# Fill and gate splits of a fused attention and mixture-of-experts kernel: relu and scale of the sums' input on ScalarE, constant rows shared out by engine, the gate splits one operation a step

## What is computed

```python
# attention: 2 batches, 8 heads, 576 positions, 64 columns a head
scores = scale * q @ k.T
cum = cumsum(maximum(s, 0))                    # s: one value per position and head
scores = where(causal, -1e9, scores + minimum(-(cum_i - cum_j), 0))
attn = exp(scores - max(scores)); attn /= sum(attn) + 1e-9
x = attn @ v                                   # then 1152 tokens of 512 values
logits = x @ w_gate; noise_scale = log1p(exp(x @ w_noise))   # stage 2: choose 2 of 8
out[mask] += weight * (maximum(x[mask] @ w1[e], 0) @ w2[e])
P = exp(x @ moe2_w_gate - max); 8 rounds of balancing        # stage 3: all 8 experts, dense
out += P[:, e] * (maximum(x @ w1[e], 0) @ w2[e])
```

## Time and profile before

| what | us |
|---|---|
| median of 3 runs (lowest to highest) | 1201.5 (1199.59 to 1203.03) |
| the profiled execution | 1204.84 |
| its span, from first to last instruction | 1203.1 |
| mean granted clock of TensorE in it | 0.993 |

### The profile page before, as it was taken

How to read it: one execution, slowest core, us unless ns; L and a number is a source line. 1 busy time by engine, 2 the same in 40 slices (tenths; PEclk the granted TensorE clock), 3 DMA queues, 4 the chain that set the end, 5 groups by cost and what they waited for, 6 DMA issues and landing times.

```text
span 1203.1 us, 20068 instructions
## 1 busy us (share of the span) xinstructions
PE 1188.2 (99%) x7085; PEld 1062.0 (88%) x7085; DVE 697.3 (58%) x1584; ACT 426.4 (35%) x918; POOL 254.8 (21%) x303
## 2 busy tenths in 40 slices
PE   8999999999999999999999999999999999999998
PEld 6999888888888888889889899899899898898997
DVE  6664775554444451657566575575574675665753
ACT  7675344444344241224123232242241241332320
POOL 8767111111111456201001011011010010110110
PEclk9998999999999999999999999999999999999999
DMA  7770654444455420013120220210211201202102
GB/s 179 182 173 4 246 179 153 155 150 153 180 180 203 161 61 1 1 36 106 36 71 6 64 70 0 70 40 30 70 35 35 70 24 46 70 0 70 35 1 78
DMA packets 40230, 102.81 MB, mean 85 GB/s; under 512 B 4750, under 2 KB 23694, under 8 KB 38010
## 3 DMA queue, kind: packets, MB, share of 16 engines
q1 hardware_dynamic: 33722, 85.70, 22.7%
q0 software_dynamic: 3360, 11.01, 3.0%
q10 hardware_dynamic: 3104, 5.54, 1.4%
HBM read 87.82 MB, written 10.30 MB: 82 GB/s over the span
## 4 chain that ended last, share of the span: by engine, by line
PE 95%; DVE 2%; ACT 1%; DMA 1%; issue 1%; POOL 0%; DVEq 0%; POOLq 0%
PE bank L1164 10%; PE bank L1163 10%; PE bank L1162 9%; PE bank L1118 9%; PE bank L1116 9%; PE bank L1117 9%; PE bank L940 5%; PE bank L942 5%; PE bank L941 5%; PE bank L922 5%; PE bank L924 4%; PE bank L923 4%; PE bank L847 3%; PE bank L828 1%; PE bank L792 1%; PE bank L829 1%
## 5 line engine op out<-in xcount | busy, mean ns | idle before, releaser
L1164 PE MATMUL bank<-part2h,partl 128*128 128x512 f32 x504 | 198.6, 394 | 0.0
L1163 PE MATMUL bank<-part2l,parth 128*128 128x512 f32 x504 | 197.6, 392 | 0.0
L761 POOL TENSOR_TENSOR part2l<-raw_part,part2h 128x512 fp32r<-128x512 f32 x56 | 72.4, 1293 | 589.9 <-ACT part2h L1414 589.9
L1162 PE MATMUL bank<-part2h,parth 128*128 128x512 f32 x504 | 195.7, 388 | 0.0
L1886 DVE SCALAR_TENSOR_TENSOR x_sb<-bank,share_now,x_sb 128x512 f32<-128x512 f32 x126 | 94.1, 747 | 159.5 <-PE bank L1164 159.5
L1118 PE MATMUL bank<-x_forms,forml 128*128 128x288 f32 x448 | 132.1, 295 | 0.0
L1116 PE MATMUL bank<-x_forms,formh 128*128 128x288 f32 x448 | 131.9, 294 | 0.0
L1117 PE MATMUL bank<-x_forms,formh 128*128 128x288 f32 x448 | 131.8, 294 | 0.0
L1565 DVE SCALAR_TENSOR_TENSOR hl<-bank,hh 128x336 fp32r<-128x336 f32 (+1 forms) x88 | 45.7, 519 | 131.5 <-ACT hh L1291 131.3
L922 PE MATMUL bank<-xTh,w1h 128*128 128x336 f32 (+1 forms) x352 | 115.9, 329 | 0.7 <-DVE xTl L1545 0.5
L923 PE MATMUL bank<-xTl,w1h 128*128 128x336 f32 (+1 forms) x352 | 113.9, 324 | 0.0
(11 more groups left out here) (244 smaller groups left out, 2464.2 us busy)
## 6 DMA issues: line engine op xcount, KB each, us to landing
raw<-in_w SPq DMA_DIRECT2D x15, 2048.0 KB, 7.7
raw_part<-in_w1b SPq DMA_DIRECT2D x14, 1024.0 KB, 6.0
raw_part<-in_w2b SPq DMA_DIRECT2D x14, 1024.0 KB, 6.1
k_raw<-in_kT SPq DMA_DIRECT2D x16, 288.0 KB, 5.3
y_dram<-x_sb ACTq DMA_DIRECT2D x16, 256.0 KB, 4.4
q_raw<-in_qT SPq DMA_DIRECT2D x8, 288.0 KB, 5.0
q_two<-w2l SPq DMA_DIRECT2D x8, 288.0 KB, 5.8
x_dram<-x_sb SPq DMA_DIRECT2D x1, 2304.0 KB, 9.2
```

The lines of the kernel that those rows point to most:

```text
L1162: pe.matmul(dst, parth[:, l, ts], part2h[:, l, :], start=(l == 0), stop=False)
L1163: pe.matmul(dst, parth[:, l, ts], part2l[:, l, :], start=False, stop=False)
L1164: mm = pe.matmul(dst, partl[:, l, ts], part2h[:, l, :], start=False, stop=(l == FL - 1))
```

## The change

- Sums' input: relu and scale move from DVE (line 1455) to ACT, right behind the rounding of the identity; DVE's scan waits for a new semaphore `s_positive`.
- Constant rows: POOL fills the first two slots of k_top, and all of q_top's second, for whose ones it waits until ACT has written q_top's first; ACT writes q_top's first only. The third slots are filled by DVE inside its loop, half a slot a step in steps 0 to 3, and the two rows of ones in step 4. POOL's memset in step 4 is gone.
- `rinv`'s first filling on DVE moves from ahead of the sums to step -1.
- Fillers on PE: five of 256 columns instead of three of 512 ahead of the loop, and 128 columns instead of 256 in the nine steps before step -4.
- Gate splits: the six operations of step 60 are spread over steps 57, 58, 59, 62, 63 and 64.

```diff
-        WARM_UPS = 3
+        WARM_UPS = 5
...
-        W1_LOW_AT, EARLY_AT, GATES_AT = ALL - 4 * DC, ALL - ST, 60
+        W1_LOW_AT, EARLY_AT, GATES_AT = ALL - 4 * DC, ALL - ST, (57, 58, 59, 62, 63, 64)
...
-            for w in range(HEADS_RING):
+            for w in range(2):
                 pool.memset(k_top[w][HD:P, :].bitcast(F32), 1.0).then_inc(aug_ready, 1)
-            pool.memset(q_top[2][HD:P, :].bitcast(F32), 0.0).then_inc(q_rows_clear, 1)
+            pool.memset(q_top[1][HD:P, :].bitcast(F32), 0.0).then_inc(q_rows_clear, 1)
+            pool.wait_ge(q_rows_clear, 1)
+            pool.wait_ge(q_rows_ready, 1)
+            pool.memset(q_top[1][HD:HD + 2, :].bitcast(F32), 1.0).then_inc(q_rows_ready, 1)
...
             for k in range(-LOW_AHEAD, ALL):
-                if k == LAST_ROWS_AT:
-                    pool.wait_ge(q_rows_clear, 1)
-                    pool.wait_ge(q_rows_ready, 2)
-                    pool.memset(q_top[2][HD:HD + 2, :].bitcast(F32), 1.0).then_inc(q_rows_ready, 1)
...
             for _ in range(WARM_UPS):
-                keep_warm(BANK)
+                keep_warm(BANK // 2)
             for k in range(-ROUGH_AHEAD, ALL):
                 if k + ROUGH_AHEAD < ALL:
                     rough(k + ROUGH_AHEAD)
                 if k < 0:
-                    keep_warm(BANK // 2 if k < -SCORES_AHEAD else P)
+                    keep_warm(P)
...
             act.copy(ident_r[:], ident[:]).then_inc(ident_rounded, 1)
+            act.wait_ge(s_loaded, 32)
+            act.activation(cum_p[0:CUM_END, :], cum_s[0:CUM_END, :], ACT.Relu, scale=SQRT_D).then_inc(s_positive, 1)
             act.wait_ge(const_ready, 6)
             act.wait_ge(first_rows, 1)
-            for w in range(2):
-                act.activation(q_top[w][HD:P, 0:S], causal[HD:P, 0:S], ACT.Relu, bias=row_ones[HD:P, 0:1], scale=0.0)
-                act.activation(q_top[w][HD:P, S:N], causal[HD:P, 0:S], ACT.Relu, bias=row_ones[HD:P, 0:1], scale=0.0).then_inc(q_rows_ready, 1)
+            act.activation(q_top[0][HD:P, 0:S], causal[HD:P, 0:S], ACT.Relu, bias=row_ones[HD:P, 0:1], scale=0.0)
+            act.activation(q_top[0][HD:P, S:N], causal[HD:P, 0:S], ACT.Relu, bias=row_ones[HD:P, 0:1], scale=0.0).then_inc(q_rows_ready, 1)
...
-            link(v.tensor_copy(rinv[:].rearrange("p a b -> p (a b)"), ones[:, 0:2 * STEPS]))
-            v.wait_ge(s_loaded, 32)
-            link(v.tensor_scalar(cum_p[0:CUM_END, :], cum_s[0:CUM_END, :], 0.0, SQRT_D, ALU.max, ALU.mult))
+            v.wait_ge(s_positive, 1)
...
-            def split_gates():
-                v.wait_ge(gates_loaded, 48)
-                for which, (cn, c0, g0) in enumerate(((2 * E, 0, 0), (E, 2 * E, 4 * E))):
-                    high, low = gate_w[:, :, g0:g0 + cn], gate_w[:, :, g0 + cn:g0 + 2 * cn]
+            def split_gates(step):
+                which, part = divmod(step, 3)
+                cn, c0, g0 = ((2 * E, 0, 0), (E, 2 * E, 4 * E))[which]
+                high, low = gate_w[:, :, g0:g0 + cn], gate_w[:, :, g0 + cn:g0 + 2 * cn]
+                if step == 0:
+                    v.wait_ge(gates_loaded, 48)
+                if part == 0:
                     link(v.tensor_copy(high, gates[:, :, c0:c0 + cn]))
+                elif part == 1:
                     link(v.tensor_tensor(low, gates[:, :, c0:c0 + cn], high.bitcast(F32), ALU.subtract))
-
+                else:
                     link(v.tensor_tensor(fold[which][:], ident[0:2 * cn, 0:cn], ident[0:2 * cn, cn:2 * cn], ALU.add))
...
+            def last_rows(k):
+                cols = slice(k % 2 * S, (k % 2 + 1) * S)
+                if k == 0:
+                    v.wait_ge(aug_ready, 3)
+                if k < 2:
+                    ones_row = v.memset(k_top[2][HD:P, cols].bitcast(F32), 1.0)
+                    if k == 1:
+                        ones_row.then_inc(aug_ready, 1)
+                elif k < 4:
+                    link(v.memset(q_top[2][HD:P, cols].bitcast(F32), 0.0))
+                else:
+                    v.wait_ge(q_rows_ready, 2)
+                    v.memset(q_top[2][HD:HD + 2, :].bitcast(F32), 1.0).then_inc(q_rows_ready, 1)
...
-                if k == GATES_AT:
-                    split_gates()
+                if k == -1:
+                    link(v.tensor_copy(rinv[:].rearrange("p a b -> p (a b)"), ones[:, 0:2 * STEPS]))
+                if 0 <= k < STEPS:
+                    last_rows(k)
+                if k in GATES_AT:
+                    split_gates(GATES_AT.index(k))
```

More of the change, by code:

```diff
@@ L204, in build @@
         s_loaded = sem("s_loaded")
+        s_positive = sem("s_positive")
         cum_summed = sem("cum_summed")
@@ L388, in build @@
         CUM_ROWS = slice(FIRST_ROWS, CUM_END)
-        SECOND_LATER, LAST_ROWS_AT = 2, 4
+        SECOND_LATER = 2
         FIRST_LOWS = (0, 1, 4, 5, 2, 3, 6, 7)
@@ L1516, in token_low @@
                                 xTh[:, :, ts].bitcast(F32), ALU.subtract).then_inc(st.xTl_ready, 1)
-            def split_gates():
-                v.wait_ge(gates_loaded, 48)
-                for which, (cn, c0, g0) in enumerate(((2 * E, 0, 0), (E, 2 * E, 4 * E))):
-                    high, low = gate_w[:, :, g0:g0 + cn], gate_w[:, :, g0 + cn:g0 + 2 * cn]
+            def split_gates(step):
[5 more added lines that the diff above has]
+                if part == 0:
                     link(v.tensor_copy(high, gates[:, :, c0:c0 + cn]))
+                elif part == 1:
                     link(v.tensor_tensor(low, gates[:, :, c0:c0 + cn], high.bitcast(F32), ALU.subtract))
+                else:
                     link(v.tensor_tensor(fold[which][:], ident[0:2 * cn, 0:cn], ident[0:2 * cn, cn:2 * cn], ALU.add))
-                assert count[0] == GATES_SPLIT, count[0]
+                assert step < 5 or count[0] == GATES_SPLIT, count[0]
+            def last_rows(k):
[11 more added lines that the diff above has]
+                    v.memset(q_top[2][HD:HD + 2, :].bitcast(F32), 1.0).then_inc(q_rows_ready, 1)
             for k in range(-ROUGH_AHEAD, ALL):
@@ L1908, in _ @@
             far_half(E - 2, 1, False)
-GATES_SPLIT = 5 + 6
+GATES_SPLIT = 6 + 6
 def kernel(q, k, v, s, moe_w_gate, moe_w_noise, moe_noise, moe_w1, moe_w2, moe2_w_gate, moe2_w1, moe2_w2):
```

## The result

| kernel | median of the runs (lowest to highest), us | profiled execution, us | its span | mean granted clock in it |
|---|---|---|---|---|
| before | 1200.62 (1198.13 to 1207.29), 22 runs | 1204.84 | 1203.1 | 0.993 |
| changed | 1205.63 (1203.02 to 1208.98), 22 runs | 1203.89 | 1202.2 | 0.994 |

The changed kernel is slower by the ratio 1.0035, with a 95% interval of 1.0024 to 1.0046, which is 4.2 us (2.9 to 5.5). The forecast was 1197.1 us, faster by 4.4. The time lies above the stated range.

The account below looks back on a forecast made before the run. TensorE (PE), busy in 99% of the span, was taken to bound the kernel. From a median of 1201.5 us, 0.9 (fill), 1.1 (gate stall) and 2.4 (half the low-clock spell) were taken off, giving 1197.1; range 1194.2 to 1201.3.

Parts of the forecast that it names:

- SP's new wait: SP's queue: load_cum(2) waits for k_top's third slot until about 20, double_k(2) behind it; cost 0, at worst 1 us.
- DVE's memsets: DVE in steps 0 to 4: half a slot 0.6 us, two rows 1.2; cost 0, each maximum having over 1 us of cover.
- The sign that was named: Steps 0 to 7: the prediction is wrong if PE waits for DVE there.
- The sums' input: Fill: relu on ACT at 3.1 lets the first rough product start at 7.5 instead of 9.10, 1.6 us earlier.
- How much of it lasts: Fill: rough(5) starts some 0.5 us earlier, not 1.6, its small row standing behind the last load and landing at 12.1.
- The fillers: From rough(5) to the first scores: four fillers shrink, by at most 0.9 us; 0.4 taken.
- rival (c): Fill: PE's 1.5 us wait ahead of rough(5) drops the clock, costing 4.8 us; time 1204.3 to 1206, chance 0.07.
- The gate splits: Around 97 us: spreading them removes PE's full stall of 1.09 us, bounds 0.6 and 1.3.
- The sum: Whole kernel: median 1201.5 - 0.9 - 1.1 - 2.4 = 1197.1 us, for the fill, gate stall and half the low-clock spell.
- rival (b): Transfer queue eats the fill's gain, SP's and DVE's waits take 0.3, gate stall gives 0.8; 1201.0 us, chance 0.08.

Follow-up runs that it names:

- e12: Changed kernel with SP's load of head 2's sums' rows moved behind double_k(2), run again on another chip; 1199.54 us against 1200.45 before, ratio 0.9984.
- e11: The changed kernel as it is, run again on another chip; 1204.46 us against 1200.45 of the kernel before, ratio 1.0039.
- e6: Kernel before, with SP made to wait for the sixteenth row maximum ahead of head 2's load of sums' rows; 1209.30 us against 1203.67, ratio 1.0060.
- e4: Changed kernel with eight fillers of 128 columns on PE in its wait ahead of rough(20); 1204.52 us, ratio 1.0005 to the kernel before.
- e2: Changed kernel with SP's load of head 2's sums' rows moved behind double_k(2); 1200.28 us against 1203.09 of the kernel before, ratio 0.9968.
- e9: On e2, head 1's second copy of k (288 KB) issued behind the sums' rows instead of ahead; 1196.93 us against 1200.45 before, ratio 0.9965.
- e7: On e2, ScalarE's queue issues both transfers of the second batch's sums' rows instead of SP's; 1203.78 us against 1203.67 before, ratio 0.9994.
- e10: On e9, the fillers of the kernel before (three of 512 columns, then 256); 1197.60 us against 1200.45 before, ratio 0.9974.
- e3: Changed kernel with the third slots' constant rows on GpSimd again, DVE's loop without them; 1200.89 us, ratio 0.9984 to the kernel before.
- e1: Kernel before with only the gate splits spread over six steps; 1201.21 us against 1203.09, ratio 0.9977.
- e5: Changed kernel with the fillers of the kernel before (three of 512 columns, then 256); 1206.55 us against 1203.67 before, ratio 1.0015.
- e8: On e2, the fillers of the kernel before; 1202.75 us against 1203.67 of the kernel before, ratio 0.9988.

## Why the prediction was wrong, step by step

- **The step that failed** is the term for SP's new wait. The prediction put it as "Behind it stand v of heads 1 and 2 and double_k(2), which is needed in step 7 (about 27): 0, at worst 1". The queue behind the wait was named rightly, and the price was wrong. Moving the load behind double_k(2) gets 4.9 us back on one chip (e12 against e11), and e6 adds only a wait, a longer one, and loses 7.2. Two terms were missed. First, the time needed was compared with the issue and not with the landing: double_k(2) was issued at 24.58 before and landed at 27.7, and rough(20) started at 27.84. A transfer whose landing PE already waits for has no slack. I had the step's date and not the transfer's. Secondly, behind the 1.4 us that this added to PE's way came a stretch at half clock that cost 4.7 us more (10.2 us long; e4 is without it), though the price of the clock stood in the prediction's own text, for another stall.
- **DVE's memsets:** nearly right at 0. They took 0.54, not 0.6, the two rows 1.02 (1.2 forecast). The maximum of tile 18 began 1.6 us after its product was there; the transfer hid that in the changed kernel, and in e2 PE waited 0.29 us for it. The sign that was named, PE waiting for DVE in steps 0 to 7, thus showed, at a small price.
- **The sums' input:** right as far as it goes. Relu took 0.68 (0.7 forecast), the scan began at 4.04 (3.9), rough(0) at 7.36 (7.5). I had read the copy of rinv as waiting for GpSimd. In its new place it took 0.42 instead of 1.12, and it ended at 20.37, right behind a GpSimd operation that ended at 20.33, as before at 4.51 behind one that ended at 4.47. That fits the reading; no run tests it alone.
- **How much of it lasts:** forecast 0.5 us at rough(5), measured 0.06. The mechanism, bytes ahead of a small row, was right (e9), the landing was put at 12.1 and was about 12.5, and the reason given, the order in one queue, was too narrow (e7).
- **The fillers:** right where the clock held. From rough(5) to the first scores it took 3.11 us in e11 against 3.47 before (0.4 forecast), and e9 against e10 agrees with 0.34. In the first profile after it took 4.21. What came there was the mechanism of rival (c), which had a chance of 0.07: PE idle for 1.91 us ahead of rough(5), at half clock from 12.7 to 16.1, the first scores at 16.80 instead of 16.12. The point from which it decides was named, more idle time than the 1.19 us that the clock had survived, and so was the wait that exceeds it, 1.5 us. By its own numbers the prediction should have given this rival much more than 0.07 (further on, 0.06). Its price was too high: 0.7 us from rough(5) to rough(10) in the first profile, not 4.8. The low clock lasted 3.4 us there and not 10.2, and it cost less for each microsecond in the fill: in e3, with 10.1 us of it, rough(5) to rough(15) took 12.22 us against 9.10 before, so 3.1 more.
- **The gate splits:** right. The stall is gone, and in the two profiles the stretch gives 6.0, where 5.9 was forecast. On the median I had taken 3.5, half of the spell; e1 gives 2.8 (0.6 to 4.8), and e6 shows an execution in which the stall is there and the spell is not. That exactly half of it was taken was a guess.
- **The sum:** -4.4 was forecast, +4.2 came. Of these 8.6 us the wait ahead of rough(20) with its clock is 5 to 8 (e11 against e12; ratios of the changed kernel against e2, on two chips). The rest is the fill, where 0.9 was counted as gain, and 0.7 at the gate splits. In the first profile the clock had turned the fill's gain into a loss of 0.7 at rough(10); in e11 a gain of 0.2 was left there. As a cross-check, 6.8 us lost up to rough(25) in the profile less the 2.8 of e1 make 4.0, near the 4.2 measured. Rival (c) had 1204.3 to 1206 for the time, and 1205.6 was measured; that agreement is luck, since its price was for the fill and most of the loss came at rough(20), behind a wait that rival (b) had priced, together with DVE's, at 0.3.

## What to carry to other kernels

When a wait is put in front of a transfer, list what stands behind it in that queue, and for each entry compare the landing, not the issue, with the moment at which the consumer starts; where the consumer starts right at the landing, each tenth of a microsecond goes through. A stall of over 1 us on TensorE has to be priced together with the clock that may fall behind it, which here cost over three times what the wait had added (4.7 against 1.4 us); where the wait can't be avoided, a few fillers in it saved the larger part. A small transfer that was issued earlier gained nothing while large ones were under way, and putting off a load that is needed late did more for it than another queue.

## What the runs showed of the hardware

- Another queue did not pass the loads: the row of 576 values issued at 7.91 from ScalarE's queue was there for PE only at 13.1 (e7), and issued at 7.73 with 288 KB less ahead of it, at 11.35 (e9).
- Whether the clock fell went with the idle time in these profiles, but not strictly. Ahead of rough(5) it fell behind 1.60 to 2.24 us of idle time (the first profile after, e2, e3, e4, e5, e7, e12) and not behind 0.24 to 0.95 (e8, e9, e10, e11). Ahead of rough(20) it fell behind each idle time of 1.48 to 3.05 us (e11, the first profile after, e5, e6). Behind the gate splits it fell after 1.09 us (before) and not after 1.12 (e6).
- The granted clock of the views does not tell all of the first 12 us: in e11 it is 1.00 from 8 to 9 us, with a product at 8.55 that took 0.77 us, as one at half clock, and not 0.48. The mean granted clock of that run, 0.991, holds 20.4 us at half clock, and the views have all of these after 28 us, so it leaves such a stretch out too.
- The low clock after a stall varies from execution to execution. Behind the same wait ahead of rough(20) it lasted 10.2 us in one profile of the changed kernel and 13.7 in the other; behind the wait ahead of rough(5) it was 3.4 in e2 and 10.1 in e3. The Trainium skill ("TensorE: Matmul & The Clock Gate", "What's actually happening") calls the monitor free-running against the kernel; these differences between like stretches agree with that.
- The mean granted clock of a run goes with its time. On one chip the kernel before took 1198.8 us on average in its 5 runs at 1.000 and 1205.0 in its 5 runs at 0.994. As an estimate from these numbers, the missing 0.006 are 2 x 0.006 x 1200 = 14.4 us at half clock, which cost 6.2 us, so 0.43 us each; the prediction's 1 - 1/1.89 is 0.47, and the fill of e3 gives 3.1 / 10.1 = 0.31. e9 was at 1.000 in 5 of 11 runs and took 1196.2 in them, 2.6 us less than before at the same clock. Not all of the low clock is the attention's: the profiles of before and of e11 have two short stretches besides, in 140 to 145 and in 465 to 470 us (0.66 on average over each 5 us), where the change does nothing, and the first profile after has neither.
